# A fused attention, MLP and mixture of experts on one core: the first expert's tiles run into the MLP, scales made later, the general path first

## The reference, cut to what matters

```python
# attention: B=2, H=8, S=768, D=64; n_global=8, n_local=96
scores = q @ k.T / sqrt(D) + bias          # bias: -slope * distance
scores = where(is_global | is_local, scores, -1e9)
x = softmax(scores) @ v                    # -> x: 1536 tokens x 512
# MLP: 512 -> 2048 -> 512
h = x @ w_in;  g = h * tanh(log1p(exp(min(h, 20))));  x2 = g @ w_out
# mixture, E=4: 512 -> 1024 -> 512 for each expert
p = domain_probs / (domain_probs.sum(-1) + 1e-9)
out = sum_e p[:, e] * (relu(x2 @ w1[e]) @ w2[e])
```

## Time and profile before

| | us |
|---|---|
| median of 3 runs | 983.41 (980.81 to 983.61) |
| the profiled execution | 979.82 |
| its span, first to last instruction | 978.0 |
| PE busy | 896.2 |
| DVE busy | 527.5 |
| ACT busy | 330.8 |
| POOL busy | 265.4 |

### The profile page before, as it was taken

The page is one execution under the profiler, slowest core; times in us unless marked ns, Lnnn a source line. Parts: engine busy times, 40 slices in busy tenths (PEclk is TensorE's granted clock), DMA queues, the critical chain, the costliest instruction groups (busy, mean ns, idle before and its releaser), DMA issues.

```text
span 978.0 us, 12849 instructions
## 1 busy us (share of the span) xinstructions
PE 896.2 (92%) x4880; PEld 461.7 (47%) x4880; DVE 527.5 (54%) x1020; ACT 330.8 (34%) x703; POOL 265.4 (27%) x206
## 2 busy tenths in 40 slices
PE   4868887799999997997599999999999999999998
PEld 3757766544444443443244444444444444444443
DVE  7866685699989899797353222432224413122221
ACT  4758976455454555454201010010101101010010
POOL 1169404922222233222005800049000291000000
PEclk9888998899999998999799999999999999999999
DMA  9811610040000002000200040000400000000001
GB/s 186 246 37 34 212 28 3 4 172 1 1 6 1 4 1 86 4 1 1 88 1 6 15 156 1 1 5 0 172 1 1 5 0 0 1 11 32 22 21 43
DMA packets 52580, 39.30 MB, mean 40 GB/s; under 512 B 41136, under 2 KB 42288, under 8 KB 52016
## 3 DMA queue, kind: packets, MB, share of 16 engines
q1 hardware_dynamic: 52528, 38.64, 13.7%
HBM read 35.48 MB, written 3.15 MB: 40 GB/s over the span
## 4 chain that ended last, share of the span: by engine, by line
PE 60%; DVE 20%; DMA 9%; ACT 7%; issue 3%; POOL 1%; SPq 0%; DVEq 0%; ACTq 0%
PE bank L566 52%; PE bank L589 5%; DMA max<-sc 4%; DMA rows<-max 4%; DVE tmp L1201 2%; DVE tmp L1203 2%; ACT tmp L736 2%; DVE tmp L1219 2%; DVE xT L1217 2%; ACT tmp L766 2%; DVE wpieces L916 1%; DVE tmp L1207 1%; DVE hid L1211 1%; DVE tmp L1072 1%; DVE tmp L965 1%
## 5 line engine op out<-in xcount | busy, mean ns | idle before, releaser
L855 ACT ACTIVATE hid<-bank 128x512 f16<-128x512 f32 x96 | 57.0, 596 | 418.7 <-PE bank L566 418.7
L566 PE MATMUL bank<-xT,wA 128*128 128x512 f16 (+1 forms) x864 | 194.8, 379 | 2.9 <-DVE hid L1258 1.5
L589 PE MATMUL bank<-hid,wB 128*128 128x512 f16 x576 | 137.8, 391 | 12.9 <-DVE hid L1211 5.5
L1258 DVE SCALAR_TENSOR_TENSOR hid<-bank,hid 128x512 f16<-128x512 f32 x96 | 65.2, 689 | 149.7 <-ACT hid L855 149.7
L566 PEld LDWEIGHTS bank<-xT,wA 128*128 128x128 f16 x864 | 84.5, 98 | 105.2 <-DVE hid L1258 2.0
L659 POOL TENSOR_SCALAR stage<-stage,sc 128x1024 f32<-128x1024 f32 x40 | 44.8, 1120 | 307.7 <-DVEq L1193 250.0
L566 PE MATMUL bank<-xT,wB 128*128 x576 | 125.5, 379 | 1.4 <-DVE hid L1258 1.4
L566 PE MATMUL bank<-wA,hid 128*128 128x512 f16 x576 | 125.3, 379 | 0.0
L566 PE MATMUL bank<-wB,hid 128*128 128x512 f16 x576 | 125.3, 379 | 0.0
L696 POOL TENSOR_TENSOR tmp<-tmp 128x512 f32<-128x512 f32 x48 | 70.1, 1461 | 188.6 <-DVE tmp L1219 188.6
L1271 DVE SCALAR_TENSOR_TENSOR acc<-bank,pg,acc 128x512 f32 (+1 forms) x36 | 27.0, 751 | 137.0 <-PE bank L566 137.0
(11 more groups left out here) (105 smaller groups left out, 993.7 us busy)
## 6 DMA issues: line engine op xcount, KB each, us to landing
stage<-in_moe_w SPq DMA_DIRECT2D x8, 2048.0 KB, 9.4
stage<-in_moe_w_in SPq DMA_DIRECT2D x1, 4096.0 KB, 14.4
stage<-in_moe_w_out SPq DMA_DIRECT2D x1, 4096.0 KB, 15.2
hid<-in_q SPq DMA_DIRECT2D x16, 192.0 KB, 4.1
hid<-in_k SPq DMA_DIRECT2D x16, 192.0 KB, 4.1
xT<-in_v SPq DMA_DIRECT2D x8, 384.0 KB, 6.4
out_y<-acc SPq DMA_DIRECT2D x12, 256.0 KB, 2.0
rows<-max SPq DMA_DIRECT2D x4, 128.0 KB, 4.0
```

Of the source, the lines that this page charges most:

```text
L566: last = pe.matmul(dst, lhs(c, a), rhs(c, b), start=(c == 0 and n == 0), stop=(c == chunks - 1 and n == 2))
L589: last = pe.matmul(psum(4 + d), w_out_s[:, a, f, d * P:(d + 1) * P], hv[:, T % RING, b, :], start=(f == 0 and n == 0), stop=(f == FT - 1 a ...
L855: act.activation(hv[:, f, 0, :], psum(f % 4), ACT.Relu).then_inc(h_hi, 1)
L1258: dve.scalar_tensor_tensor(hv[:, f, 1, :], psum(f % 4), 0.0, hv[:, f, 0, :], ALU.max, ALU.subtract).then_inc(h_ready, 1)
```

## The change

In words:

- **Flow.** The drain of the MLP (T = 48 to 51) now has `expert_first(0, 0, T - 48)` in it: PE puts the first four tiles of expert 0, group 0, between the last second products. ACT and DVE have `expert_high` and `expert_low` at the same places. For this x2 is kept in the last tiles of `acc` (`y32`), no longer in the first.
- **Last x2.** The maximum, the scale and the halves of group 2's x2 are made during group 0 and group 1 of expert 0.
- **Scales.** Those of w_in and w_out come at units 29 and 83 (were 25 and 79); expert 0's maxima at every second step from T = 6, its scale at T = 25 (was 19); its pieces at T = 32, 34, 39, 41 and 48 to 51 (were 31 to 34 and 48 to 51); x2's scale 7 steps after the group's end (was 5), its high halves 8 (was 6). The scales of experts 1 to 3 are made in group 1, behind its tiles (were at the end of group 0).
- **Branch.** The general attention path stands first in the program and the banded one after it.
- **Loops.** ACT and DVE have the mixture's groups written out; PE keeps its loop except for expert 0, group 0.

```diff
@@ -205,7 +205,7 @@
...
-        y32 = acc[:, 0:DC * GN].rearrange("p (c n) -> p c n", c=DC)
+        y32 = acc[:, (NT - GT) * DM:].rearrange("p (c n) -> p c n", c=DC)
...
@@ -286,13 +287,14 @@
...
-        W0_MAX = 8
-        W0_SCALE = 19
-        W0_HIGH = 31
-        X2_SCALE = 5
-        X2_HIGH = 6
+        W0_MAX = [6 + 2 * c for c in range(PIECES)]
+        W0_SCALE = 25
+        W0_HIGH = [32, 34, 39, 41] + [STEPS + c for c in range(PIECES // 2)]
+        W0_LOW = [T + 1 for T in W0_HIGH[:PIECES // 2]] + W0_HIGH[PIECES // 2:]
+        X2_SCALE = 7
+        X2_HIGH = 8
...
@@ -360,10 +362,10 @@
...
-            with eng.If(banded == 1):
+            with eng.If(banded == 0):
+                run(False)
+            with eng.Else():
...
-            with eng.Else():
-                run(False)
...
@@ -433,9 +435,9 @@
             sp.wait_ge(w0_lo, PIECES // 2)
             load_w1(1)
             share_x2_max(1)
-            share_x2_max(2)
             sp.wait_ge(w0_lo, PIECES)
             load_w2(1)
+            share_x2_max(2)
             share_weights_max(3)
             for e in range(2, E):
                 sp.wait_ge(w_split, 1 + e)
...
@@ -595,46 +597,58 @@
...
+            def expert_first(e, g, f):
+                w1_s, _ = expert(e)
+                cols = bass.ds(g * GN, GN)
+                if e == 0 and f == 0:
+                    if isinstance(g, int):
+                        pe.wait_ge(w0_lo, PIECES // 2)
+                    pe.wait_ge(x_ready, XN + DC * g + DC)
+                if f >= 4:
+                    pe.wait_ge(f_ready, ET * (NG * e + g) + f - 3)
+                elif isinstance(g, int):
+                    pe.wait_ge(b_ready, STEPS + f - 3)
+                split_product(psum(f % 4), lambda c, s: w1_s[:, s, c, f * P:(f + 1) * P],
+                              lambda c, s: xv[:, c, s, cols], DC).then_inc(h_psum, 1)
+            def expert_group(e, g, begun=0):
+                _, w2_s = expert(e)
+                for f in range(begun, ET):
+                    expert_first(e, g, f)
+                if isinstance(g, int):
+                    pe.wait_ge(x2_taken, DC * NG)
+                    pe.wait_ge(w0_lo, PIECES)
+                for j in range(GT):
+                    pe.wait_ge(y_added, NT * e + GT * g + j + 1)
+                    split_product(psum(4 + j), lambda c, s: hv[:, c, s, j * P:(j + 1) * P],
+                                  lambda c, s: w2_s[:, s, c, :], ET,
+                                  (lambda c: pe.wait_ge(f_ready, ET * (NG * e + g) + c + 1)) if j == 0 else None,
+                                  ).then_inc(y_psum, 1)
...
+                else:
+                    expert_first(0, 0, T - STEPS)
...
-            for e in range(E):
-                w1_s, w2_s = expert(e)
-                if e == 0:
-                    pe.wait_ge(w0_lo, PIECES // 2)
-                else:
-                    pe.wait_ge(w_split, 2 + e)
+            expert_group(0, 0, LAG)
+            with pe.Fori(1, NG) as g:
+                expert_group(0, g)
+            for e in range(1, E):
+                pe.wait_ge(w_split, 2 + e)
...
-                    n = STEPS + ET * NG * e
-                    cols = bass.ds(g * GN, GN)
-                    if e == 0:
-                        pe.wait_ge(x_ready, XN + DC * g + DC)
-                    for f in range(ET):
-                        if f >= 4:
-                            pe.wait_ge(h_ready, n + ET * g + f - 3)
-                        split_product(psum(f % 4), lambda c, s: w1_s[:, s, c, f * P:(f + 1) * P],
-                                      lambda c, s: xv[:, c, s, cols], DC).then_inc(h_psum, 1)
-                    if e == 0:
-                        pe.wait_ge(x2_taken, DC * NG)
-                        pe.wait_ge(w0_lo, PIECES)
-                    for j in range(GT):
-                        pe.wait_ge(y_added, NT * e + GT * g + j + 1)
-                        split_product(psum(4 + j), lambda c, s: hv[:, c, s, j * P:(j + 1) * P],
-                                      lambda c, s: w2_s[:, s, c, :], ET,
-                                      (lambda c: pe.wait_ge(h_ready, n + ET * g + c + 1)) if j == 0 else None,
-                                      ).then_inc(y_psum, 1)
+                    expert_group(e, g)
...
+            def expert_high(e, g, f):
+                act.wait_ge(h_psum, STEPS + ET * (NG * e + g) + f + 1)
+                if (e, g) == (0, 0):
+                    act.wait_ge(l2_done, STEPS - RING + f + 1)
+                act.activation(hv[:, f, 0, :], psum(f % 4), ACT.Relu).then_inc(f_hi, 1)
...
@@ -840,23 +863,18 @@
...
-                if W0_HIGH <= T < W0_HIGH + PIECES // 2:
-                    expert_0_high(T - W0_HIGH)
-                if T >= STEPS:
-                    expert_0_high(PIECES // 2 + T - STEPS)
+                if T in W0_HIGH:
+                    expert_0_high(W0_HIGH.index(T))
...
-            for c in range(DC):
-                x2_high(NG - 1, c)
-            def expert_group(e, g):
-                n = STEPS + ET * NG * e
-                for f in range(ET):
-                    act.wait_ge(h_psum, n + ET * g + f + 1)
-                    act.activation(hv[:, f, 0, :], psum(f % 4), ACT.Relu).then_inc(h_hi, 1)
+            for f in range(LAG, ET):
+                expert_high(0, 0, f)
...
-                with act.Fori(0, NG) as g:
-                    expert_group(e, g)
+                for g in range(0 if e else 1, NG):
+                    for f in range(ET):
+                        expert_high(e, g, f)
+                        if (e, g) == (0, 1) and f >= ET - DC:
+                            x2_high(NG - 1, f - ET + DC)
...
@@ -1021,7 +1039,7 @@
...
-                scales = {0: 2 * UNITS + 1 if banded else 2 * UNITS - 1, 1: (6 if banded else 7) * UNITS + 7}
+                scales = {0: 2 * UNITS + (5 if banded else -1), 1: 7 * UNITS + (-1 if banded else 7)}
...
@@ -1231,52 +1257,50 @@
...
-                if W0_MAX <= T < W0_MAX + PIECES:
-                    weights_part(2, T - W0_MAX)
-                elif T == W0_MAX + PIECES:
+                if T in W0_MAX:
+                    weights_part(2, W0_MAX.index(T))
+                if T == W0_MAX[-1] + 1:
...
-                elif T == W0_SCALE:
+                if T == W0_SCALE:
...
-                elif W0_HIGH < T <= W0_HIGH + PIECES // 2:
-                    expert_0_low(T - W0_HIGH - 1)
-                elif T >= STEPS:
-                    expert_0_low(PIECES // 2 + T - STEPS)
-            for c in range(DC):
-                x2_max(NG - 1, c)
-            x2_scale(NG - 1)
-            for c in range(DC):
-                x2_low(NG - 1, c)
-            def expert_group(e, g):
-                n = STEPS + ET * NG * e
-                share = pr[:].rearrange("p (t e) -> p e t", e=E)[:, e, bass.ds(g * GT, GT)]
+                if T in W0_LOW:
+                    expert_0_low(W0_LOW.index(T))
+            def expert_group(e, g, begun=0):
+                share = pr[:].rearrange("p (t e) -> p e t", e=E)[:, e, g * GT:(g + 1) * GT]
...
-                dve.tensor_scalar(pg[:], share, inv_g[:, bass.ds(g, 1)], inv_e[:, e % 2:e % 2 + 1],
+                dve.tensor_scalar(pg[:], share, inv_g[:, g:g + 1], inv_e[:, e % 2:e % 2 + 1],
...
-                for f in range(ET):
-                    dve.wait_ge(h_hi, n + ET * g + f + 1)
-                    dve.scalar_tensor_tensor(hv[:, f, 1, :], psum(f % 4), 0.0, hv[:, f, 0, :],
-                                             ALU.max, ALU.subtract).then_inc(h_ready, 1)
+                for f in range(begun, ET):
+                    expert_low(e, g, f)
+                    if (e, g) == (0, 0):
+                        x2_max(NG - 1, f - begun)
+                    if (e, g) == (0, 1) and f >= ET - DC:
+                        x2_low(NG - 1, f - ET + DC)
+                if g == 1 and e + 1 < E:
+                    expert_scales(e + 1)
...
-                    if isinstance(g, int) and e + 1 < E:
+                    if g == 0 and e + 1 < E:
...
-                    y = acc[:, bass.ds((g * GT + j) * DM, DM)]
+                    y = acc[:, (g * GT + j) * DM:(g * GT + j + 1) * DM]
...
+                if g == 0 and e + 1 < E:
+                    weights_max(3 + e)
+                if (e, g) == (0, 0):
+                    x2_scale(NG - 1)
+            expert_group(0, 0, LAG)
...
-                expert_group(e, 0)
-                if e + 1 < E:
-                    weights_max(3 + e)
-                    expert_scales(e + 1)
-                with dve.Fori(1, NG) as g:
+                for g in range(0 if e else 1, NG):
```

29 lines of the change are left out of this document (19 added, 10 removed).

## The result

| | before | changed |
|---|---|---|
| median of the timed runs | 982.27 us (980.81 to 983.61, 4 runs) | 955.88 us (954.70 to 957.35, 4 runs) |
| profiled execution | 979.82 us, span 978.0 | 954.70 us, span 952.9 |

The ratio is 0.9732, 95% interval 0.9710 to 0.9755: the changed kernel is 2.7% faster. The forecast was 954 (952.0 on the scale of the profiled execution).

The account below looks back on a forecast made before the run. PE, busy 92%, was taken to bound the kernel from the MLP on, DVE's stops the attention. Terms -9.3 + 0.7 - 6.2 - 19.5 - 4.4 + 10.9 = -27.8 took 979.8 to 952.0, 954 on medians; range 940 to 966.

Parts of the forecast that it names:

- Scales four units later: Attention: later w_in and w_out scales remove DVE's two waits for rows of maxima; -9.3 us, bounds 7 to 11.
- about 3 us of cover are left: Head of the MLP: POOL's wB is still done about 3 us before PE comes for it.
- General path first: Attention: the jump moves from the end (2.6 us back) to the start (3.3 us); +0.7 us, bounds 0 and 7.
- Pieces spread, x2 scales later: MLP at T = 36: PE's hole and slower products, 7.8 us, shrink to a hole of 1.6; -6.2 us.
- First tiles without a break: From MLP to expert 0: its first products cover the waits for hidden tiles; -19.5 us, other bound -10.
- Experts' scales: Mixture: scales made after group 1's tiles end DVE's three waits, which reached PE as 4.4; -4.4 us.
- What the new order adds: MLP, T = 43: SP's order delays x2 group 1's maxima, PE waits for tile 42; +10.9 us, bounds 2.7 and 14.3.
- t0: MLP, T = 42: the end of expert 0's fourth piece; the row of maxima was taken to land 18 us after.
- rival with the hidden stop: MLP, T = 43: the new stop for x2's maxima hardly shows; 943 us, chance 0.22.
- the gains come short: T = 36 hole stays (+6.2), maxima row at upper bound (+3.4), or jump (+3.7): any two 960 to 968; chance 0.17.

Follow-up runs that it names:

- SyncE's other order: The changed kernel with share_x2_max(1) on SP ahead of the wait for the fourth low piece and load_w1(1); 945.92 us, ratio 0.9668.
- the last kernel: All four edits on the changed kernel: maxima row first on SyncE, banded path first, x's last turn at T=1, w_out's maxima paired, scale at unit 79; 945.64 us.
- the kernel of 940.79 us: The changed kernel with row of maxima first on SyncE, banded path first and last turn of x at T = 1, not 2; 940.79 us, ratio 0.9591.

## Why the prediction was right, and where not

- **Scales four units later: -9.3 forecast.** The mechanism holds for the attention: the wait of 5.41 at the first scale is 0.80 (at 76.53), and the second is gone. With the scales back the attention is 10.6 longer, within the bounds 7 to 11. The step that failed is "about 3 us of cover are left", on two counts. First, the split. The prediction moved it "by about 1 us at most with the start" and "by 4 to the front with the first scale". The 4 came (it ends at 195.8, and at 200.1 with the scales back), by way of the second scale and not of the first. But the later start moved it by 4.0 to the back (191.8 with the banded path first), so it ended as before (195.8 and 196.0). By the prediction's own terms the cover would have been 2.9 + 4 - 1 = 5.9, not 3. Second, what stands behind the split. The prediction took GpSimd's part to be wB alone, and the multiply for tile 0, queued behind it, had no cover at all once PE came 10.6 us earlier. 6.3 us were lost there.
- **General path first: +0.7.** PE's start came 4.4 later and VectorE's first table 4.6 (12.87; forecast 3.3), the gap behind the attention shrank by 2.6 (forecast 2.6), and part of the late start was made good on the way. At the turn of x it is +0.6 against the run with the banded path first, and 0.0 between the kernel before and the run with the scales back (183.49 in both): both within the spread of this place. In the span it was +2.1, through the split. By the Trainium skill (Runtime: NRT & Kernel Launch, Instruction fetch mechanics) a taken branch whose target isn't in the loaded window waits until its page is fetched. The runs agree: each order of the two paths has one gap of "issue" more, at the start (first matmul at 12.85, and at 8.50 with data as the releaser) or at the end (3.31).
- **Pieces spread, x2 scales later: -6.2.** -5.9, with the hole of 1.6 that was forecast. The run with the pieces back shows that only 3.7 of it is due to them.
- **First tiles without a break: -19.5.** -19.6; 8.3 from the interleaving, 11.3 with the moved x2 scale, by difference.
- **Experts' scales: -4.4.** -5.0 up to the end of the span; PE has no wait left in the mixture. Not tested by itself.
- **What the new order adds: +10.9.** +9.7: a hole of 7.93 for 8.3, a slower product of 1.6 for 2.6. The row came 16.6 us after t0, not 18. The rival with the hidden stop (943) was wrong, and it is what SyncE's other order gives (943.0 of span).

The forecast had 27.8 off the span and the trace has 25.1. Of the 6.3 us lost at the head of the MLP, 2.0 were made good because PE was 10.6 ahead at the turn of x and not 8.6, 1.2 by the smaller stop at T = 43, and 0.4 by the other three terms together. That the total came within 2.7 us is thus in part luck: the largest error was covered by smaller ones with the other sign. Two more workings of the prediction don't come out. The profiled execution was 3.6 under the median, so 952.0 would be 955.6 on the scale of medians, and the forecast said 954 (measured 955.88). In the rival "the gains come short" two of the three additions give 7.1 to 9.9 on 952, so 959 to 962, and not 960 to 968.

## What to carry to other kernels

When a stage gets shorter, list for the first work behind it every engine that it passes through, and ask of each what is queued ahead: that its data is ready is half of the question, since the engine may still be at the work that made the data. Look at what a moved step releases as closely as at what it costs: the fourth piece was cheap where it went, but what SyncE did after it was not. On a queue that only issues transfers, the small one with a reader waiting goes ahead of the large one with none.

## What the runs showed of the hardware

VectorE's instructions beside GpSimd's take much longer, but only some of them. Three lines of VectorE in the changed kernel, each 48 times (duration in ns: least, median, longest):

```profile
L1225 DVE TENSOR_SCALAR tmp<-tmp x48: 414/587/1497, 181.5 to 444.7; 128x512 f32<-128x512 f32 x48
...
L1227 DVE SCALAR_TENSOR_TENSOR tmp<-tmp x48: 691/693/2485, 182.3 to 446.3; 128x512 f32<-128x512 f32 x48
...
L1231 DVE SCALAR_TENSOR_TENSOR tmp<-bank,tmp x48: 691/691/692, 183.7 to 447.1; 128x512 f32<-128x512 f32 x48
```

L1227 and L1231 are the same instruction at the same size (the first adds and multiplies, the second multiplies twice). L1227 reads both inputs from SBUF and took up to 2.49 us; L1231 reads one from PSUM and never took over 0.692, in the middle of one of GpSimd's long instructions too (L1231 from 188.59, GpSimd's L678 from 188.09 to 190.54).

The Trainium skill (SBUF — State Buffer, Terms) says that VectorE and GpSimd share a port pair that one of them holds for a whole instruction while the other is blocked, and (GPSIMD Engine Reference, Specifications) that this concerns VectorE's instructions with two SBUF inputs or in a 2-port performance mode. This trace agrees for the two inputs: the 2.48 of L1227 at 193.83 end 0.5 us behind GpSimd's 2.17 of L678 from 193.60, a little less than the 0.69 that L1227 takes alone. L1225 has one SBUF input and took up to 1.50 for 0.41; whether it ran in such a mode the trace doesn't say.

The hole of 8.74 us also costs behind its end. Windows of PE in the changed kernel (start and end, length, busy, granted clock, DMA share, GB/s):

```profile
195.00:200.00 5.00, 0.00 (x0) 0.68 0.57 201
200.00:204.00 4.00, 0.72 (x2) 0.50 1.01 373
204.00:208.00 4.00, 4.00 (x13) 0.62 1.02 381
208.00:212.00 4.00, 4.00 (x20) 1.00 0.12 46
```

and of the last kernel, which has no hole there:

```profile
195.00:200.00 5.00, 5.00 (x25) 1.00 1.02 390
```

0.50 is the lower level of 1.2 GHz. It was granted while PE stood idle and on into the first product, which took 4.61 for 2.75; the DMA engines were full in both kernels (shares of 1.01 and 1.02), so they are not the cause. A short hole can go either way: after 2.14 us at T = 36 the product took 2.75 in the kernel of 940.79 us, after 2.17 it took 4.44 in the one with all four edits. At the head of the MLP waits of 3.3 and 1.42 us were followed by a first product of 2.76 in the kernel before and of 4.72 in the one with the banded path first. What decides stays open.
